# Order of VectorE's work in the first tile of a fused attention, gated product and normalised product kernel

## The reference, cut to what matters

```python
# attention: q, k, v are (4, 8, 576, 64)
out_up    = repeat(softmax_attention(mean4(q), mean4(k), mean4(v)), 4)   # "pooled", 144 positions
out_local = softmax(where(|i - j| < 4, q @ k.T / 8, -1e9)) @ v           # "local", 7 neighbours
x = (out_up + out_local) as (2304 tokens, 512)
# gated product
y = ((x @ w_a) * (x @ w_b)) @ w_out                                      # 512 -> 1536 -> 512
# second product, with a softmax gate and a layer norm over 1024 columns
h = y @ w_in;  ln = layer_norm(h * softmax(h)) * g_ln;  out = ln @ w_out2
```

## Time and profile before

| | us |
|---|---|
| median of 3 runs (lowest, highest) | 793.74 (793.35, 793.88) |
| the profiled execution's own time | 793.58 |
| its span, first to last instruction | 791.4 |
| PE busy | 759.7 (96%) |
| DVE busy | 560.9 (71%) |
| ACT busy | 298.2 (38%) |
| POOL busy | 214.7 (27%) |

### The profile page before, as it was taken

How to read it: one execution, slowest core, us unless ns; L and a number is a source line. 1 busy time by engine, 2 the same in 40 slices (tenths; PEclk the granted TensorE clock), 3 DMA queues, 4 the chain that set the end, 5 groups by cost and what they waited for, 6 DMA issues and landing times.

```text
span 791.4 us, 12269 instructions
## 1 busy us (share of the span) xinstructions
PE 759.7 (96%) x4440; PEld 695.3 (88%) x4440; DVE 560.9 (71%) x975; ACT 298.2 (38%) x819; POOL 214.7 (27%) x260
## 2 busy tenths in 40 slices
PE   6878889899999999999999999999999999999998
PEld 5767888799999999999999999999988888888886
DVE  4579999979979787778777876022467666666663
ACT  3443655454353525344524424224322212222222
POOL 2467977638414421041001111121100000000000
PEclk9999999999999999999999999999999999999999
DMA  9999958584887586683956433637121011011011
GB/s 189 192 237 221 217 117 258 199 259 149 265 244 243 169 244 183 186 203 106 256 163 188 149 107 110 205 102 228 39 66 54 27 54 54 27 55 53 27 41 41
DMA packets 96652, 117.27 MB, mean 148 GB/s; under 512 B 19921, under 2 KB 59603, under 8 KB 96593
## 3 DMA queue, kind: packets, MB, share of 16 engines
q1 hardware_dynamic: 81872, 106.98, 49.0%
q10 hardware_dynamic: 14721, 9.51, 4.2%
HBM read 95.62 MB, written 20.84 MB: 147 GB/s over the span
## 4 chain that ended last, share of the span: by engine, by line
PE 79%; DVE 0%; ACT 0%; issue 0%; DVEq 0%
PE psum L851 25%; PE psum L853 24%; PE psum L852 24%; PE psum L963 2%; PE psum L807 1%; PE psum L787 1%; PE psum L797 1%; PE psum L818 1%; PE psum L769 0%; DVE acc L1470 0%; DVE accT L1479 0%; ACT p_pool L1059 0%; ACT out_sb L1262 0%; ACT out_d L1077 0%; DVE ab_f L1381 0%
## 5 line engine op out<-in xcount | busy, mean ns | idle before, releaser
L851 PE MATMUL psum<-x_hi,w_hi 128*128 128x384 f32 x576 | 199.5, 346 | 2.3 <-DVE x_lo L1375 1.4
L853 PE MATMUL psum<-x_hi,w_lo 128*128 128x384 f32 x576 | 194.1, 337 | 0.0
L852 PE MATMUL psum<-x_lo,w_hi 128*128 128x384 f32 x576 | 193.9, 337 | 0.0
L851 PEld LDWEIGHTS psum<-x_hi,w_hi 128*128 128x128 f32 x576 | 109.2, 190 | 6.5 <-issue 4.6
L852 PEld LDWEIGHTS psum<-x_lo,w_hi 128*128 128x128 f32 x576 | 109.4, 190 | 0.0
L853 PEld LDWEIGHTS psum<-x_hi,w_lo 128*128 128x128 f32 x576 | 109.0, 189 | 0.0
L1381 DVE TENSOR_TENSOR ab_f<-psum,a_sb 128x384 f32<-128x384 f32 x72 | 39.8, 553 | 90.9 <-PE psum L853 62.0
L851 PE MATMUL psum<-ab_hi,wo_hi 128*128 128x384 f32 x288 | 99.8, 346 | 3.3 <-issue 3.3
L853 PE MATMUL psum<-ab_hi,wo_lo 128*128 128x384 f32 x288 | 96.6, 335 | 0.0
L852 PE MATMUL psum<-ab_lo,wo_hi 128*128 128x384 f32 x288 | 96.4, 335 | 0.0
L1689 POOL TENSOR_TENSOR raw<-raw 96x256 f32<-96x256 f32 x60 | 55.5, 951 | 123.2 <-DMA raw<-in_q 59.2
(11 more groups left out here) (147 smaller groups left out, 1420.0 us busy)
## 6 DMA issues: line engine op xcount, KB each, us to landing
wo_hi<-wo_hi_scratch SPq DMA_DIRECT2D x53, 256.0 KB, 2.7
wo_lo<-wo_lo_scratch SPq DMA_DIRECT2D x53, 256.0 KB, 3.1
k_u<-in_k SPq DMA_DIRECT2D x11, 576.0 KB
v_u<-in_v SPq DMA_DIRECT2D x11, 576.0 KB
k_u<-in_k SPq DMA_DIRECT2D x17, 288.0 KB
v_u<-in_v SPq DMA_DIRECT2D x17, 288.0 KB
wo_raw<-in_moe_w_out SPq DMA_DIRECT2D x19, 256.0 KB, 4.9
raw<-in_v SPq DMA_DIRECT2D x8, 576.0 KB, 6.7
```

Of the source, the lines that this page charges most:

```text
L851: mm(dst, wh, xh, start=first, stop=False, skip_group_check=not check)
L852: mm(dst, wh, xl, start=False, stop=False, skip_group_check=not check)
L853: last = mm(dst, wl, xh, start=False, stop=end, skip_group_check=not check)
```

## The change

In tile 0, and only there, `gate` and `ab_low` of DVE are moved into `between`, behind the slot's part of a pooled job and ahead of its local step: `ab_low(j)` in slot 3j, `gate(j+1)` in slot 3j+1. No instruction is added or removed, and the other engines' queues are as they were.

```diff
             def between(m, n):
                 for i, since in jobs_at(m, n):
                     if since == 1:
                         pooled_max(i)
                     if since == TURN:
                         pooled_inverse(i)
+
+                if m == 0 and n % 3 == 1:
+                    gate(n // 3 + 1)
+                if m == 0 and n % 3 == 0:
+                    ab_low(n // 3)
                 local_steps(m, n)
                 if n in turns_at(m):
                     x_low(m + 1, turns_at(m)[n])
...
                     between(m, 3 * j)
-                    if m < LOW_BY_POOL:
+                    if 0 < m < LOW_BY_POOL:
                         ab_low(g)
                     between(m, 3 * j + 1)
-                    if g + 1 < FC * TILES:
+                    if m > 0 and g + 1 < FC * TILES:
                         gate(g + 1)
                     between(m, 3 * j + 2)
```

## The result

The changed kernel is slower: its ratio to the kernel before is 1.0071, 95% interval 1.0047 to 1.0094, or +5.6 us (3.7 to 7.5) on 793.6. The medians are 800.21 and 793.62, of 8 runs each. The forecast was +3.6. The profiled execution took 802.01 us, the longest of the eight: it tells where the time lies better than how much it is.

The account below looks back on a forecast made before the run. PE bounds the whole, but in tile 0 PE waits for DVE's full queue. Terms 0 + 0.55 + 2.0 + 1.45 + 0.47 = 4.5, less 0.9, gave +3.6 on 793.6: 797.2 us, forecast case 795.4 to 799.5 (0.58), range 792.3 to 800.6.

Parts of the forecast that it names:

- The waits: In tile 0 DVE would wait for PE or ACT before gates 3, 4, 8 and 10: 0.75, 3.7, 2.0, 1.2 us.
- PE's 2.87: PE's early wait for the pooled attention copy in tile 0, 2.87 us plus some 1.3 of slowed clock, would go.
- slots 0 to 7: Start of tile 0: early gate -0.5, POOL contention +1.0, gate 3 wait +0.75, old wait -1.3, +0.1: about 0.
- slots 8 to 10: DVE waits 3.7 us at gate 4, product and add then take 3.6: +0.55, bounds -1.1 and +3.1.
- slot 21 to step 9 in slot 23: Gate 8 loses its cover while PE turns `accT`: DVE waits 2.0 us, bounds 1.6 and 2.3.
- to the end of slot 28: Slots 24 to 28: DVE waits 0.25 at `ab_low(9)` and 1.2 at gate 10: +1.45, bounds 0.3 and 2.3.
- to the last `x_lo`: Slot 33: `ab_low(11)` now stands ahead of `x_low` instead of behind it: +0.47 us.
- relief: POOL clears work while DVE idles, so one or two fewer DVE operations are slowed late in tile 0: -0.9 us.
- The rival of one POOL instruction at most: DVE loses no more than 0.7 us at a time to POOL, `pool_den` of slot 8 takes 0.9: 795.1, chance 0.05.
- Faster (791.5): DVE reaches `pool_den` of slot 8 before POOL's instructions, ahead of 84.1, so it costs 0.2: 791.5 us, chance 0.14.
- no change (794): DVE's idle time is just what POOL would have taken from it: 794 us, chance 0.11.
- Much slower (800.3): Slot 10's add is blocked its full 5.48 us after DVE's 3.7 wait, again at slot 12: 800.3, chance 0.12.

Follow-up runs that it names:

- e1: Changed kernel with only the twelve gates of tile 0 ahead of the local steps, the remainders (`ab_low`) left behind them: 797.27 us, ratio 1.0054.
- e5: Kernel before with gate 4 alone moved ahead of its local step: 795.08 us, ratio 1.0026.
- e4: Kernel before with gate 1 alone moved ahead of its local step: 792.85 us, ratio 0.9992.
- e8: Changed kernel with POOL's subtractions for the remainders of the weights and `w_out` replaced by memsets to zero: 785.62 us, ratio 0.9898.
- e9: Kernel before with POOL's subtractions for the remainders of the weights and `w_out` replaced by memsets to zero: 783.42 us, ratio 0.9861.
- e7: Kernel before with gate 1 ahead of its local step and `x_low` ahead of it in slots 32 and 33 of tile 0: 793.17 us, ratio 0.9990.
- e12: As e7, with END of the second unit in slot 30 instead of 31: 792.84 us, ratio 1.0006 to the kernel before.
- e10: Kernel before with `x_low` alone moved ahead of the local step in slots 32 and 33 of tile 0: 792.63 us, ratio 0.9989.
- e6: Kernel before with gate 8 alone moved ahead of its local step: 794.52 us, ratio 1.0012.

## Why the prediction was right

*Where the bound lies.* Right as far as the runs reach: e1 and e5 lengthen DVE's queue and lose time, the delay at the last down product of tile 0 (6.4 us) is found unchanged one and two tiles on (6.3), and the time behind the last `x_lo` differs by at most 3 us between kernels whose `x_lo` differs by 8.6. That PE's early idle time would be worth nothing was not tested, as no run with subtractions takes it away (e4). The reading of the earlier trace rows was loose: DVE is at 9 in the slices 10, 11 and 13 too, but PE is at 9 there and has no holes, so nothing hangs on it.

*The waits.* Forecast at gates 3, 4, 8 and 10: 0.75, 3.7, 2.0 and 1.2. Found: 0.95, 3.79, 2.12, and 1.25 at gate 9 instead of 10; I had left gate 9 a margin of 0.1. At `ab_low(0)` 0.59 against 0.7; the 0.25 at `ab_low(9)` is not there.

*The signs.* Two of those I named failed. PE's 2.87 went, but 3.18 for POOL's `w_lo` came in its place and the clock from 70 to 75 us is 0.66, lower than the 0.77 of before; I had both as gone. And PE does not wait longer than 1.43 for the last `x_lo`: it does not wait for it at all, its lost time stands before the second `accT` (3.89) and in the slow products behind. The `x_lo` itself starts at 161.95, where I had said near 160.

*The sum by stretches.* Measured from the first gate, with DVE's start of slot 8 (the second `pool_den`), of slot 11, of slot 21, of step 9 in slot 23, the end of slot 28 and the start of the last `x_lo` as marks, the changed profile minus the one before is:

| stretch | forecast | found |
|---|---|---|
| slots 0 to 7 | 0 | +4.0 |
| slots 8 to 10 | +0.55 | -1.2 |
| slots 11 to 20 | 0 | +0.9 |
| slot 21 to step 9 in slot 23 | +2.0 | +1.3 |
| to the end of slot 28 | +1.45 | +0.8 |
| to the last `x_lo` | +0.47 | +0.8 |
| relief | -0.9 | |
| sum | +3.6 | +6.5 |

*Slots 0 to 7* is the mis-sized term. There I had the early gate 1 pay for itself and POOL's extra contention at 1.0. POOL in the changed kernel, from 66 us:

```profile
68.59 2.77 POOL L1706 TENSOR_TENSOR w_lo<-w_raw,w_hi 128x256 fp32r<-128x256 f32 x4
71.32 1.41 POOL L1714 TENSOR_TENSOR wo_lo<-wo_raw,wo_hi 128x256 fp32r<-128x256 f32 x2
72.69 2.80 POOL L1706 TENSOR_TENSOR w_lo<-w_raw,w_hi 128x256 fp32r<-128x256 f32 x4
```

The early gate frees ACT for the next block's weights, POOL goes from one group to the next with no gap, and a 128x2 operation of DVE is held for 5.72 us, until 74.82, within 0.7 us of POOL's end. Before, POOL stood idle 2.8 us ahead of the second group of weights, and DVE ran:

```profile
73.14 4.48 POOL L1701 TENSOR_TENSOR w_lo<-w_raw,w_hi 128x256 fp32r<-128x256 f32 x4 [2.81 <-ACT w_hi L1117]
```

Leaving out e8 and e9, in five of the seven profiles with gate 1 early these slots take 27.9 to 28.3 us, in the two others (e7, e12) 24.0 and 24.8; of the five with gate 1 late three take 23.4 to 23.9 and two 26.2 and 27.1. So the change makes the long case likelier; one kernel can fall either way, since POOL's start hangs on a load (the one behind POOL's sums in slot 0 let it start at 58.53, against 55.65 before). *Slots 8 to 10* came out at -1.2 here. Up to the third `pool_den` (slot 15) the four subtracting kernels with gate 4 early take 50.2 to 52.2 us from the first gate, the eight others 46.1 to 50.8: the two errors are partly the same held time at another place, and +2.1 for gate 4 (e5) is the better figure than either.

*The last `x_lo`.* DVE was ready for it at 161.0 but had to wait 0.94: `accT` came late, PE had stood 3.89 us, and its next product ran at 1.2 GHz, 12 starts 0.32 apart and not 0.175, which is 1.7 us. I had PE's long wait only as a thing that goes away in slot 4, not as one that comes in slot 32.

*The same difference by kind.* DVE's idle time up to the last `x_lo` grew by 8.55 us, from 1.30 to 9.85; the forecast has 8.6 of waits less the old 1.3, so 7.3. DVE's other time shrank by 2.1, where the forecast, with 3.6 in all, has 3.7. So there was relief, of less than I took, and the waits were 1.3 longer: the 0.94 at `x_lo` and 0.21 at gate 1 are most of it.

*How much of it was luck.* By the ratio the changed kernel stands at 799.2, inside the 795.4 to 799.5 of the forecast; the median of its runs, 800.21, lies outside and next to the rival of 800.3. The waits came out nearly as walked. The size came near with +4.0 where I had 0 and -1.2 where I had +0.55, and the account of PE's early wait and clock was wrong.

*How long POOL can hold DVE.* The rival of one POOL instruction at most fell: 5.72 us spans some nine of them, and without POOL's subtractions the long operations are gone from the changed kernel (e8), though the 2.90 of e9 spans ten memsets. The Trainium skill, page "SBUF — State Buffer", section "Who interferes with whom", also says that an operation with two inputs from SBUF contends with POOL only where POOL reads; the products of q and k agree (1.00 against 1.15 us in e8, 0.96 against 1.47 in e9), as far as memsets of 0.31 us can show it. The held 128x2 operations have one input and are not of that kind.

*The other rivals.* Faster (791.5) and no change (794) fall with the interval of +3.7 to +7.5. In the one place that decides the first, `pool_den` of slot 8 came at 88.08, not ahead of POOL's weights, and took only 0.58; no wait was spared by it. Against no change speaks also that the wait at gate 4 and the held time were both paid in e5. Much slower (800.3) gave about the right time by the wrong mechanism: in slot 10 the product took 2.67 and the add 1.49, not 5.48.

Left open: how the 5.6 us divide. The single costs measured are gate 4 +2.1, gate 8 +1.0, the remainders +1.3, all gates +4.3, each with an interval of 1.2 to 1.5 us to a side. Gates and remainders add to 5.6, which fits, but the clock at the end of the tile has an unknown part in each, and gates 4 and 8 together leave 1.2 of the gates' 4.3 to the others and to the longer held time.

## What to carry over

On an engine that works through a fixed order and is the bound of a stretch, work that waits for nothing is the cover of the operations that wait. Moving a waiting operation ahead of it serves only the engine that waits for the result, and here it cost time; that it would pay where that engine is the bound is not shown by a run. Ask first which queue ends the stretch. When such a move makes a neighbour busier (here POOL, through ACT), look at what the neighbour holds up.

## What the runs showed of the hardware

- A DVE operation over 128x2 elements took 5.72 us, and 5.73 to 5.77 in e5, e7, e10 and e12, while POOL ran subtractions back to back, and 2.90 in e9 beside memsets; the same operation takes 0.15 us at 126.22 in the changed kernel. A single small operation can thus be the most expensive one of a stretch.
- With POOL's subtractions replaced by memsets the kernel before gains 11.0 us (9.0 to 13.1): twice what the change costs, and far more than any order tried here.
- After 3.89 us of waiting PE ran at 1.2 GHz, as for a while after the 2.87 us in the profile before; after waits of 1.06 and 1.43 us in the profile before it kept its full clock (the window from 155 to 160 us has 1.00). The wait alone doesn't decide: after 2.84 us at 72.31 in e6 the clock from 70 to 80 us is 1.00.
